# One core, linear attention and two feed-forward layers: attention of a chunk on TensorE in three lumps, another slot plan for the first pass, and the weights' low parts on VectorE

## The reference

```python
B, H, S, D = 4, 8, 768, 48
for t in range(S):                                  # attention, per batch and head
    cur = einsum('bhd,bhe->bhde', u[None] * kt, vt)
    y[:, :, t] = einsum('bhd,bhde->bhe', rt, state + cur)
    state = wt[:, :, :, None] * state + einsum('bhd,bhe->bhde', kt, vt)
# x: (3072 tokens, 384)
h = x @ w_in                                        # first layer, 1024 wide
e = np.exp(h - h_max)
solu = h * (e / (e.sum(-1) + 1e-9))
ln = (solu - mu) / np.sqrt(var + 1e-6) * g_ln
x = ln @ w_out
h = x @ w_in                                        # second layer, 2048 wide
out = np.maximum(0.01 * h, h) @ w_out
```

## Time and profile before

| | us |
|---|---|
| median of three runs | 834.44 |
| the profiled execution, whole | 831.91 |
| its span | 829.4 |
| PE busy | 784.7 (95%) |
| DVE busy | 511.8 (62%) |
| ACT busy | 345.0 (42%) |
| POOL busy | 208.1 (25%) |
| mean granted TensorE clock | 0.985 of full |

### The profile page before, as it was taken

The page is one execution under the profiler, slowest core; times in us unless marked ns, Lnnn a source line. Parts: engine busy times, 40 slices in busy tenths (PEclk is TensorE's granted clock), DMA queues, the critical chain, the costliest instruction groups (busy, mean ns, idle before and its releaser), DMA issues.

```text
span 829.4 us, 12139 instructions
## 1 busy us (share of the span) xinstructions
PE 784.7 (95%) x4624; PEld 739.3 (89%) x4624; DVE 511.8 (62%) x1044; ACT 345.0 (42%) x676; POOL 208.1 (25%) x226
## 2 busy tenths in 40 slices
PE   3998988789999999999999999999999999999996
PEld 2767888679999999999999999999999999999996
DVE  7774576666575766667665766666765775553332
ACT  3358354334433444434434444335333443334332
POOL 6448743423111221121221131122122122000000
PEclk9999899899999999999999999999999999999998
DMA  8940202203202302203202122103012030000000
GB/s 241 338 145 1 58 0 58 58 1 87 58 1 58 83 4 58 58 2 86 58 1 57 25 62 58 29 30 87 24 35 58 1 87 29 1 1 29 1 1 31
DMA packets 18846, 43.49 MB, mean 52 GB/s; under 512 B 2272, under 2 KB 14688, under 8 KB 18400
## 3 DMA queue, kind: packets, MB, share of 16 engines
q1 hardware_dynamic: 14736, 33.24, 15.9%
q10 hardware_dynamic: 4048, 9.44, 3.4%
HBM read 37.95 MB, written 4.72 MB: 51 GB/s over the span
## 4 chain that ended last, share of the span: by engine, by line
PE 76%; DVE 3%; ACT 2%; issue 1%; ACTq 0%
PE BANKS L1122 53%; PE MISC L1122 20%; PE BANKS L1301 2%; DVE EXP L910 1%; PE MISC L1139 1%; ACT EXP L629 1%; PE MISC L1146 1%; DVE hmax L900 1%; DVE RL L983 0%; DVE RL L981 0%; ACT RH L703 0%; DVE Rraw L974 0%; ACT Rraw L697 0%; ACT RH L701 0%; DVE nmax L903 0%
## 5 line engine op out<-in xcount | busy, mean ns | idle before, releaser
L697 ACT ACTIVATE Rraw<-BANKS 128x384 f32<-128x384 f32 x128 | 62.9, 491 | 254.9 <-PE BANKS L1122 254.7
L974 DVE TENSOR_TENSOR Rraw<-BANKS,Rraw 128x384 f32<-128x384 f32 x128 | 71.3, 557 | 139.7 <-ACT Rraw L697 139.4
L1122 PE MATMUL BANKS<-RH,W4H 128*128 128x384 f32 x384 | 139.9, 364 | 0.9 <-DVE RL L981 0.8
L1122 PE MATMUL BANKS<-X2H,W3H 128*128 128x384 f32 x384 | 132.4, 345 | 0.7 <-DVE X2L L989 0.7
L1122 PE MATMUL BANKS<-RH,W4L 128*128 128x384 f32 x384 | 130.1, 339 | 0.0
L1122 PE MATMUL BANKS<-RL,W4H 128*128 128x384 f32 x384 | 130.1, 339 | 0.0
L1122 PE MATMUL BANKS<-X2L,W3H 128*128 128x384 f32 x384 | 130.0, 339 | 0.0
L1122 PE MATMUL BANKS<-X2H,W3L 128*128 128x384 f32 x384 | 130.0, 338 | 0.0
L701 ACT ACTIVATE RH<-Rraw 128x384 fp32r<-128x384 f32 x128 | 67.2, 525 | 73.3 <-DVE Rraw L974 73.3
L981 DVE TENSOR_TENSOR RL<-Rraw,RH 128x384 fp32r<-128x384 f32 x128 | 79.1, 618 | 23.7 <-ACT RH L701 23.7
L486 POOL TENSOR_TENSOR ke<-att 112x512 f32<-112x512 f32 x24 | 29.5, 1229 | 245.1 <-DVE att L841 245.1
(11 more groups left out here) (138 smaller groups left out, 1519.8 us busy)
## 6 DMA issues: line engine op xcount, KB each, us to landing
att<-rkw SPq DMA_DIRECT2D x48, 288.0 KB, 4.8
out<-OUT SPq DMA_DIRECT2D x8, 576.0 KB, 5.5
rtok<-r_tok SPq DMA_DIRECT2D x22, 192.0 KB, 4.4
ktok<-k_tok SPq DMA_DIRECT2D x22, 192.0 KB, 4.5
vtok<-v_tok SPq DMA_DIRECT2D x22, 192.0 KB, 4.6
W3raw<-w_in ACTq DMA_DIRECT2D x1, 3072.0 KB, 22.9
W4raw<-w_out ACTq DMA_DIRECT2D x1, 3072.0 KB, 13.9
W1raw<-w_in ACTq DMA_DIRECT2D x1, 1536.0 KB, 14.5
```

Source lines behind the costliest of these rows:

```text
L697: nc.scalar.activation(Rraw[:, fp % 2, :], PR[fp % 2][:, 0:ST], ACT.Copy, scale=0.01).then_inc(act_slope, 1)
L974: nc.vector.tensor_tensor(Rraw[:, fp % 2, :], PR[fp % 2][:, 0:ST], Rraw[:, fp % 2, :], ALU.max).then_inc(dve_relu, 1)
L1122: return nc.tensor.matmul(dst, lhsT, rhs, start=start, stop=stop, skip_group_check=True)
```

## The change

Five things change.

1. On PE a chunk's attention is in three lumps: at s=3 all four pairs' scores and then the key transposes; at s=5 all four pairs' `attend` and the fresh state; at s=7 the output's transposes as before. The scores of four pairs now take two whole banks, and the key transposes go to the bank of `Y` (`keys_of`).
2. DVE masks the scores in two instructions of 128x512 in place of four of 128x256, both at s=4, with `own_sums` behind them. ACT takes the keys at s=4 instead of s=1.
3. The 28 slots of the first 16 steps follow a table: seven in the first three steps, then a chunk in each cycle of five steps (2, 2, 1, 2, 1).
4. All 24 low parts move from POOL to DVE: eight in the opening, sixteen in the first pass. ACT's high parts in the opening are spread anew, and POOL's small items move by a slot or two.
5. W1's load is issued by SP before chunk 1's tokens; W3's and W2's loads are issued later by ACT. In the last step of an M1 stage DVE does `step_lo` ahead of the slot.

```diff
+def opening_slots(f):
+    ahead = ((1, 2, 3, 4), (5, 6), (7,))
+    cycle = ((8, 9), (10, 11), (12,), (13, 14), (15,))
+    after = ahead[f] if f < 3 else [s + (f - 3) // 5 * SLOTS for s in cycle[(f - 3) % 5]]
+    return [slot_of(CPS * SLOTS + s) for s in after]
...
+            load_T(0, 1)
+            sp.dma_start(w1, w_in1.rearrange("(k p) n -> p k n", p=128)).then_inc(ld_w[0], 16)
+            load_tok(0, 1)
...
 # POOL
-            def low_part(w, g):
...
-                    if s == 2:
+                    if s == 1 and 0 < m % CPB < CPB - 1 and not ahead:
+                        decayed_state(b, m)
+                    if s == 2 and not ahead:
                         own_token(b, m, 0)
...
-                    if s == 4:
+                    if s == 5:
                         own_token(b, m, 1)
-                        if 0 < m % CPB < CPB - 1:
-                            decayed_state(b, m)
...
 # ACT
-                    if s == 1:
+                    if s == 4:
                         take_keys(b, m)
...
             take_ln(1)
+            high_part(3, 0)
             normalise(0, 2)
             part_heads(0, 3)
+            high_part(3, 1)
+            take_ln(2)
+            take_range(0, 3)
+            take_x2(0, 0)
             for g in range(6, 8):
                 high_part(2, g)
...
 # DVE
-                    if s in (2, 3, 4, 5):
-                        mask(b, m, s - 2)
-                    if s == 3:
+                    if s == 4:
+                        mask(b, m, 0)
+                        mask(b, m, 2)
                         own_sums(b, m)
...
+            def low_part(w, g):
+                dve.wait_ge(split_hi[w], g + 1)
...
+                nc.vector.tensor_tensor(group(los[w], w, g), group(raws[w], w, g),
+                                        group(his[w], w, g).bitcast(F32), ALU.subtract).then_inc(split_lo[w], 1)
...
+                    if opening(b, kind, so):
+                        if f == 0:
+                            low_part(0, 3)
+                        if f % 2 == 0 and 4 + f // 2 < GROUPS[2]:
+                            low_part(2, 4 + f // 2)
+                        if f % 2 == 1 and 1 + f // 2 < GROUPS[3]:
+                            low_part(3, 1 + f // 2)
+                        if f % 2 == 0 and 0 < f // 2 <= GROUPS[1]:
+                            low_part(1, f // 2 - 1)
...
 # PE
-                if s == 1:
...
-                    transpose_keys(b, m)
-                if 2 <= s <= 5:
...
-                if 3 <= s <= 6:
...
+                if s == 3:
+                    wait(pe, dve_he, chunks(b, m, 2))
+                    scores(b, m)
                     transpose_keys(b, m)
+                if s == 5:
+                    wait_tok(pe, b, m)
+                    wait(pe, act_keT, chunks(b, m, 1, 1))
+                    for a in range(PAIRS):
+                        wait(pe, dve_masked, chunks(b, m, PAIRS, a // 2 * 2 + 2))
+                        attend(b, m, a).then_inc(pe_y, 1)
+                    if m % CPB < CPB - 1:
+                        fresh_state(b, m)
```

More of the change, by code:

```diff
@@ L74, in batch_steps @@
     for k, so, f, fp in out:
[L75 to L79, removed]
-    return listed
+        listed.append((k, so, f, fp, opening_slots(f) if opening and fp <= STEPS else [slot_of(fp + LEAD)]))
+    return listed
+def opening_slots(f):
[3 more added lines that the diff above has]
+    return [slot_of(CPS * SLOTS + s) for s in after]
 def first_steps():
@@ L228, in build @@
         XT = MISC[:, 512:512 + MODEL]
-        SCO = [MISC[:, 512 * (i + 1):512 * (i + 1) + 2 * CH] for i in range(2)]
+        KT = MISC[:, 0:PAIRS * PD]
         TB = MISC[:, FF1:FF1 + 512]
@@ L776, in _ @@
                 high_part(2, g)
+            for g in range(3):
+                high_part(0, g)
             take_x(0, 2)
@@ L994, in run @@
                     m, s = items[0]
-                    item(b, m, s)
+                    last_rows = kind == "M1" and f == F1 - 1
+                    if last_rows:
+                        step_lo(b, kind, f, fp)
+                    for at, t in items:
+                        item(b, at, t)
                     if kind == "M2":
@@ L1062, in _ @@
             row_max(0, 2)
+            for g in range(2, 4):
+                low_part(2, g)
             times_exp(0, 2)
@@ L1199, in attend @@
                     c = (2 * a + h) * D
-                    last = mm(Y[:, c:c + D], masked(b, m)[:, at, h, :], tokens(2, b, m)[:, c:c + D], not inter and a == 0 and h == 0, True)
+                    last = mm(Y[:, c:c + D], masked(b, m)[:, a, h, :], tokens(2, b, m)[:, c:c + D], not inter and a == 0 and h == 0, True)
                 return last
@@ L1207, in fresh_state, with scores, first_scores @@
                 last.then_inc(pe_state, 1)
-            def first_scores(m, pairs):
+            def scores(b, m):
+                if m % CPB > 0 and not first(b, m):
+                    wait(pe, dve_state, states(b, m - 1))
+                for a in range(PAIRS):
+                    if first(b, m):
+                        ready = m * PAIRS + sum(n for at, n in portions(0, m) if at <= a)
+                    else:
+                        ready = chunks(b, m, PAIRS, PAIRS)
+                    wait(pe, dve_keys, ready)
+                    wait(pe, act_rb, ready * 2)
+                    mm(scores_of(b, m, a)[:, a % 2 * 2 * CH:(a % 2 + 1) * 2 * CH], keys(b, m)[:, a, :],
+                       rb[:, a, :, :].rearrange("p h t -> p (h t)"), a % 2 == 0, True).then_inc(pe_scores, 1)
+            def first_scores(m):
                 if m == 2:
                     pe.wait_ge(dve_masked, 2 * PAIRS)
-                for a in pairs:
-                    ready = m * PAIRS + sum(n for at, n in portions(0, m) if at <= a)
-                    pe.wait_ge(dve_keys, ready)
-                    pe.wait_ge(act_rb, 2 * ready)
-                    mm(scores_of(m, a)[:, a % 2 * 2 * CH:(a % 2 + 1) * 2 * CH], keys(0, m)[:, a, :],
-                       rb[:, a, :, :].rearrange("p h t -> p (h t)"), a % 2 == 0, True).then_inc(pe_scores, 1)
+                scores(0, m)
             def first_keys(m):
```

145 lines of the change are left out of this document (52 added, 93 removed).

## The result

The kernel after takes 825.38 us (median of 7 runs, 823.09 to 830.28) against 834.44 us (831.18 to 835.66): a ratio of 0.9900, 95% interval 0.9879 to 0.9922. The gain is 9.1 us where 17.4 were forecast; the time lies in the range. The profiled execution took 823.23 us, with a span of 821.3.

A forecast was written before the change was run, and what follows sets the result against it. PE was taken to bound the kernel, with 24.1 us lost to idling and clock in the first pass. Gains of 14.1 (pass), 2.4 (opening) and 1.0 (lumps) sum to 17.5, so 834.44 becomes 817 us; range 808 to 829.

The forecast's parts named there:

- the row over the rule: First pass: count RL's stall as the trace row shows it, four POOL instructions long, not one as the skill's rule says.
- Places where I expect PE to wait: First pass: list of PE's remaining waits, 7 us idle in all with 0.5 of small ones, instead of 16.8.
- (a): First pass, step 0: DVE's 8.4 us of work against PE's 6.5; PE waits about 1.5 at the transposes of s=7.
- (c): M1 stage behind the first pass: needs chunk 5's normalised rows, some 2 us late as before the change.
- (b): First pass, step 4: DVE's work ahead of chunk 4's masks; PE waits some 2 us at the lump, about 1 for chunk 5.
- the prediction's own signs: First pass: M1 transposes start at 160 to 166 us, PE idle 5 to 9 us; a pass over 95 us means wrong.
- The price of a low part: A low part on DVE in the first pass: 0.93 us from a slope, ends 0.68 and 1.87.
- a few us: First pass: by the skill's rule, low parts on DVE wait this long for POOL's token products; no row showed it.
- The rival of a DVE-bound pass: First pass: half of the 16 low parts stand ahead of something PE needs, 7.4 us come back, 824; chance 0.15.
- The opening's 2.4 us: Opening: gain of 1.3 from W1's earlier load and 1.1 from PE's wait for ACT; ends -1.5 and 4.
- 1.0 us gained: Steady stretch: fewer returns to dense work save 0.09 us each, joints inside lumps cost 0.09 each; 1.0 us taken.
- The lower end of the bounds: Steady stretch: the lumps lose 4 us, against 7.6 gained if the joints cost nothing.

The follow-up runs named there:

- e12: e9 with all low parts on POOL again, at e1's places: 821.50 us, ratio 0.9844 to the kernel before.
- e3: The kernel after, with ACT taking the keys of chunks 4 and 5 ahead of the normalised rows: 823.69 us, ratio 0.9873.
- e4: The kernel after, with the first pass's 16 low parts dealt to other steps on DVE: 824.94 us, ratio 0.9884.
- e9: e5 with the last low parts of W4 and W2 and chunk 7's scans moved on DVE to clear chunk 5's rows: 810.99 us, ratio 0.9695.
- e5: The kernel after with the changes of e3 and e4, and before's order of attention from chunk 7 on: 814.13 us, ratio 0.9763.
- e6: The kernel after, with one more 128x128 transpose ahead of each chunk's three output transposes from chunk 6 on: 830.42 us, ratio 0.9951.
- e11: The kernel after, with the key transposes ahead of the scores in the lump of s=3 from chunk 4 on: 829.91 us, ratio 0.9930.
- e7: The kernel after, with the attend lump split between s=5 and s=6 from chunk 7 on: 826.44 us, ratio 0.9904.
- e10: e9 with 28 unused transposes of the identity on PE ahead of the first scores: 810.65 us, ratio 0.9693.
- e2: The kernel before, with only its 24 low parts moved to DVE: 828.60 us, ratio 0.9941.
- e1: The kernel after, with all 24 low parts back on POOL, lumps and five-step cycles kept: 826.27 us, ratio 0.9876.
- e8: The kernel after, with 18 unused transposes of the identity on PE ahead of the first scores: 828.27 us, ratio 0.9909.

## Why the forecast was half right

**The mechanism in the first pass was right.** RL was held up by POOL's run, and with the low parts gone from POOL its longest is 0.56 us. e12 shows the same at larger size: RL ends at 122.15 us, 0.4 after the end of POOL's run at 121.73. The Trainium skill ("SBUF — State Buffer", Who interferes with whom) ties such a stall to one instruction of the other engine; here it lasted over seven of up to 1.9 us, as the earlier trace rows had shown over four. Choosing the row over the rule was right.

**The step that failed is "Places where I expect PE to wait", 7 us idle.** It was 12.0. The list of places walked through DVE's order alone. Of its places (a), the transposes of s=7, came as forecast (1.42 us), and so did (c), the late rows at the M1 stage (2.23 us, 2.2 before). In place of (b), 2 and 1 us at the masks, stood 3.8 and 2.5 us at keT, 3.3 more, and the small waits came to 2.0 us instead of 0.5. The prediction did not follow ACT's queue: the diff moved `take_keys` from s=1 to s=4, behind the normalised rows, and these hang on moments on DVE and rstd on POOL. DVE's low parts delay that chain. e3 takes the keys out of the queue and leaves just the masks' 2.1 and 0.9 us; e4 and e9 take low parts out of the chain. With both, the pass becomes 82.0 us with 3.6 idle, better than the 90.6 that the forecast came to; e9 shows that (c) was a matter of order too.

The pass itself was missed by 4.7 us: 5.0 more idle and 1.8 more clock (4.8 against 3), less some 2 of PE's own work. Three of the prediction's own signs said so: the M1 transposes start at 167.3 us and not at 160 to 166, the idle time is over 9 us, and the pass is over the 95 us that were named as wrong.

**The price of a low part was 1.2 us in the mean, not 0.93.** The groups of after's pass (the sixteenth low part, of W1, took 0.89):

```profile
L962 DVE TENSOR_TENSOR RL<-Rraw,RH 128x384 fp32r<-128x384 f32 x15 | 7.9, 529 | 0.6 <-ACT RH L689 0.6
...
L973 DVE TENSOR_TENSOR W4L<-W4raw,W4H 128x768 fp32r<-128x768 f32 x7 | 7.3, 1044 | 0.0
L973 DVE TENSOR_TENSOR W2L<-W2raw,W2H 128x768 fp32r<-128x768 f32 x4 | 5.4, 1348 | 0.0
L973 DVE TENSOR_TENSOR W3L<-W3raw,W3H 128x768 fp32r<-128x768 f32 x4 | 5.2, 1294 | 0.0
```

Twenty of after's 24 take 0.89 to 0.96, the slope's value; four take 1.58 to 2.56. The mean of the fifteen above is 17.9 / 15 = 1.19. The long ones stand beside POOL's work: in e5 one took 2.78 us, from 140.84 on, while POOL ran its end keys and token products. That agrees with the same section of the Trainium skill, which the prediction had named for it. The 0.26 x 15 = 3.9 us were called "a few us" and stood outside the sum. That DVE's busy time in the pass came out at the forecast's 74.4 us is luck: the low parts took 3.9 us more than their term, and the rest less. The rival of a DVE-bound pass came nearest in time, 824. It had DVE's order as the cause, which e4 bears out, but not the way by which that reached PE, ACT's queue.

**The opening's 2.4 us came by luck.** The profiled pair shows 2.5. The terms that the prediction lists add up to 3.3 (1.3 + 1.1 - 0.5 + 1.4), and its sum took in the first two alone. And the same opening starts the pass at 72.0, 72.3, 72.7, 72.7, 75.2, 76.7, 77.0 and 77.1 us in after, e9, e5, e6, e3, e4, e11 and e7. PE's first six fp32 products show why, in after and in e4:

```profile
20.15 2.84 PE L1133 MATMUL BANKS<-W1raw,X 128*128 128x512 f32 x6 [0.58 <-ACT X L641]
```

```profile
23.17 5.37 PE L1130 MATMUL BANKS<-W1raw,X 128*128 128x512 f32 x6 [0.58 <-ACT X L641]
```

The wait for W1's load is gone in both, as forecast. But in e4 PE's work before 28.3 us takes about twice its time, and in after only that before 15.7: value products start 0.214 us apart instead of 0.112, as they do in e10's stretch with a granted clock of 0.50. So PE is at the lower level of its clock, 1.2 GHz, until then. The windows show 1.00 there because the trace holds no record of the clock ahead of its first change, which stands at just these times. Before's profile has a third form, a fall behind the first rise:

```profile
20.00:25.00 5.00, 3.12 (x5) 1.38 (x6) 4.90 (x9) 1.74 (x5) 2.18 (x2) 0.79 1.04 416
25.00:30.00 5.00, 5.00 (x30) 3.97 (x28) 2.86 (x5) 1.43 (x3) 1.48 (x3) 0.87 1.01 406
```

That costs it (0.21 + 0.13) x 5 = 1.7 us, which after's profiled execution did not pay, so of the 2.5 us some 0.8 are left for the change (an estimate). All fourteen profiles sort by this: a whole clock from 15.7 to 17.1 us on goes with a start at 72.0 to 72.7 (after, e5, e6, e9), one fall between 22 and 36 us with 74.5 to 76.0 (before, e2, e3, e10), and the low level until 27.3 to 29.0 us with 76.3 to 77.2 (e1, e4, e7, e8, e11, e12). e9's six runs are 806.1 and 806.2, and then 811.0 to 811.4, and after's spread is 823 to 830; the same difference would make it, but no slower run of these has a profile. One profile of each kernel can't resolve a 2 us term ahead of 28 us.

**The steady stretch had the wrong sign: 1.0 us gained was forecast, 4.35 were lost** (from the first to the seventh M1 stage, 572.62 to 576.97). No product waits. Timeline of PE in after, one attend lump, and the starts of nine 384-column products from the end of another:

```profile
390.12 0.36 PE L1133 MATMUL MISC<-state,att 112*128 112x96 f32 x2
390.31 0.57 PE L1133 MATMUL MISC<-vtok,A 128*128 128x48 f32 x4
390.72 0.43 PE L1133 MATMUL MISC<-state,att 112*128 112x96 f32 x2
390.98 0.57 PE L1133 MATMUL MISC<-vtok,A 128*128 128x48 f32 x4
```

```profile
332.65 0.34 PE L1133 MATMUL BANKS<-X2H,W3H 128*128 128x384 f32 x1
...
334.24 0.34 PE L1133 MATMUL BANKS<-RH,W4H 128*128 128x384 f32 x1
```

Nine products take 1.59 us here, 176.6 ns each, where 1.56 (173.3) is what before mostly has. Sorting every start-to-start distance of the four super-chunks by what stands on its two sides gives the account (us, and the count of distances):

```
                                   before          after
behind a 384/512-column product   309.72 (1656)   309.62 (1656)
score to the next                  18.87   (96)    20.74   (96)
state to state                      3.31   (40)     5.54   (40)
value product to the next          18.75  (192)    19.84  (192)
all others (transposes, fresh)     31.60           29.39
sum                               382.24          385.12
```

The joints inside a lump cost what the term gave them: 2.2 us at the state products and 1.1 at the value products, 3.3 over 36 joints, 0.09 each. Three things are off. The returns to dense work that went are 32 and not 48, worth 32 x 0.09 = 2.9 us instead of 4.3. The slow pitch (130 of 239 groups of nine, before 39) took about that back, and no row of before that was read had warned of it. And the last small product in front of dense work hides in it: a score costs 0.215 us to the next small one but 0.027 in front of a 384-column product, so with the key transposes behind them the twelve lumps of scores cost 1.9 us more; the forecast had priced scores at nothing. The transposes gave 2.2 back, since those of the M1 stages seldom stand ahead of a score any more. The prices of the joints and of the last small product could be read from before's trace, had its distances been sorted by neighbour and not read from one pair. The lower end of the bounds, 4 us lost, was right, the value taken was not.

In sum, of the profiled executions, 823.23 is 8.8 us above the forecast's 814.4: 4.7 in the pass (95.35 against 104.7 - 14.1), 5.35 in the steady stretch, and 0.1, 0.6 and 0.6 less in the opening, the tail and around the span. With 1.7 us of the opening owed to the clock of before's profiled execution, the sum would be off by 1.6 us more.

**Open:** what sets the pitch of 173 or 177 ns. It is not the number of transposes (e6), and e7 (125 of 239) and e11 (150) moved it without ruling it. That low parts close behind it on DVE make rstd long is shown (2.01 us in after, 0.55 in e4 and in e1); how they do it is not, since in after the low part starts 0.7 us behind rstd. What moves the clock's falls between executions of the same pass is open too.

## What to carry to other kernels

When a change moves one operation down an in-order queue, follow that queue, not only the engine that gets more work: the lump waited for a copy on ACT that had been ready for its turn and stood behind somebody else's operand. Moving work to a busier engine paid nothing that could be told in one order of that engine (after against e1) and 10 us in another (e9 against e12, where the places differ too), so such a move is to be judged with its places and not by its sum. Before a gain of 2 us is put down to a change, look whether the two executions compared had the same clock. Lumping short products is no gain where each of them hides in front of a long one.

## What the runs showed of the hardware

- PE at half rate until 28.3 us (e4) or 15.7 us (after) with the same opening, where the windows print a granted clock of 1.00 for want of a record; with work ahead of it (e10) the full rate came at the scores and a granted clock of 0.50 later.
- Behind a wait of 3.1 us the clock was 0.50 from 160 to 165 us, and with the wait down to 0.8 us the super-chunk behind took 3.8 us less (e5 against e9).
- 384-column products at two pitches, 173.3 and 176.6 ns, for tens of products on end.
- One RL of 0.5 us stretched to 10.29 us by seven POOL instructions in a row (e12).
- POOL's rstd, one column, at 2.01 us with low parts on DVE behind it (after) and 0.55 without (e4).
